# A new order for four engines around TensorE's fixed list of products, in linear attention and two MLPs on one core

## The reference

```python
# q, k, v: 8 x 8 heads x 576 x 64
q_s = softmax(q, axis=-1); k_s = softmax(k, axis=2)
x = q_s @ (k_s.T @ v)                       # -> 4608 tokens x 512
h = x @ w_in                                # 512 -> 2048
x2 = (max(h, 0) + alpha * min(h, 0)) @ w_out          # 2048 -> 512
h = x2 @ w_in2                              # 512 -> 1024
sm = exp(h - max(h)) / (sum(exp(h - max(h))) + 1e-9)
solu = h * sm
ln = (solu - mean) / sqrt(var + 1e-6) * g_ln
out = ln @ w_out2                           # 1024 -> 512
```

## Time and profile before

| what | value |
|---|---|
| median of 3 runs | 1277.55 us (1273.79 to 1279.27) |
| the profiled execution's own time | 1275.84 us |
| its span | 1274.0 us |
| mean granted clock of TensorE | 0.982 |
| bytes moved | 225 MB, 177 GB/s |

### The profile page before, as it was taken

One profiled execution on the slowest core, in us unless ns is written; L12 is line 12 of the kernel. 1 busy time (PEld: TensorE's weight loads), 2 busy tenths in 40 slices (PEclk: granted clock), 3 DMA queues, 4 the chain that ended last, 5 costly groups with the idle time before them and its releaser, 6 DMA issues.

```text
span 1274.0 us, 16162 instructions
## 1 busy us (share of the span) xinstructions
PE 1207.0 (95%) x6013; PEld 992.4 (78%) x6013; DVE 938.5 (74%) x1165; ACT 539.0 (42%) x744; POOL 306.8 (24%) x233
## 2 busy tenths in 40 slices
PE   7999999999999999999999999899898998998987
PEld 6778878878788888888888888877676776776765
DVE  7858778677663658777687777847878778778773
ACT  4433443434433435344444434434534534534432
POOL 5632413314131000000000001455144244244100
PEclk8999999999999999999999999999999999999999
DMA  9787787787956463452706335964434334334243
GB/s 238 228 250 257 236 255 241 232 274 231 292 191 211 150 234 105 153 177 67 243 22 208 122 100 182 267 195 136 146 121 155 122 118 156 123 116 157 91 147 118
DMA packets 211918, 225.07 MB, mean 177 GB/s; under 512 B 63208, under 2 KB 148224, under 8 KB 211712
## 3 DMA queue, kind: packets, MB, share of 16 engines
q1 hardware_dynamic: 206064, 212.50, 52.9%
q0 software_dynamic: 5728, 11.53, 3.0%
q10 hardware_dynamic: 48, 0.01, 0.0%
HBM read 128.51 MB, written 95.48 MB: 176 GB/s over the span
## 4 chain that ended last, share of the span: by engine, by line
PE 71%; DVE 13%; issue 5%; DMA 5%; POOL 2%; SPq 2%; ACT 1%; DVEq 0%; POOLq 0%; ACTq 0%
PE ps_y L1812 8%; PE ps_y L1814 8%; PE ps_y L1813 8%; PE ps_y L1898 5%; PE ps_y L1902 5%; PE ps_y L1900 5%; DVE e L1639 5%; PE ps_y L1956 3%; PE ps_y L1957 3%; PE ps_y L1958 3%; PE ps_m L1898 3%; PE ps_m L1902 3%; PE ps_m L1900 3%; PE ps_m L1748 2%; DVE zl L1648 2%
## 5 line engine op out<-in xcount | busy, mean ns | idle before, releaser
L1812 PE MATMUL ps_y<-X,W 128*128 128x512 f32 x576 | 227.4, 395 | 0.0
L1813 PE MATMUL ps_y<-X,W 128*128 128x512 f32 x576 | 225.0, 391 | 0.0
L1814 PE MATMUL ps_y<-X,W 128*128 128x512 f32 x576 | 224.9, 391 | 0.0
L1340 DVE SCALAR_TENSOR_TENSOR gst<-gst,nslope,ps_y 128x512 f32<-128x512 f32 x144 | 104.5, 732 | 114.9 <-ACT gst L952 114.6
L952 ACT ACTIVATE gst<-ps_y 128x512 f32<-128x512 f32 x144 | 85.8, 596 | 225.2 <-PE ps_y L1814 174.4
L1956 PE MATMUL ps_y<-WO,zh 128*128 128x512 f32 x288 | 120.0, 417 | 43.5 <-DVE zl L1648 43.5
L1812 PEld LDWEIGHTS ps_y<-X,W 128*128 128x128 f32 x576 | 108.4, 188 | 23.3
L1814 PEld LDWEIGHTS ps_y<-X,W 128*128 128x128 f32 x576 | 108.5, 188 | 23.1
L1813 PEld LDWEIGHTS ps_y<-X,W 128*128 128x128 f32 x576 | 108.6, 188 | 22.0
L1898 PE MATMUL ps_y<-rh,WOc 128*128 128x512 f32 (+1 forms) x320 | 118.0, 369 | 0.0
L1900 PE MATMUL ps_y<-rl,WOc 128*128 128x512 f32 (+1 forms) x320 | 117.9, 368 | 0.0
(11 more groups left out here) (189 smaller groups left out, 2587.2 us busy)
## 6 DMA issues: line engine op xcount, KB each, us to landing
g_scratch<-gst SPq DMA_DIRECT2D x144, 256.0 KB, 3.5
RX<-g_scratch SPq DMA_DIRECT2D x36, 512.0 KB, 3.6
z_scratch<-zb SPq DMA_DIRECT2D x36, 512.0 KB, 2.7
zt<-z_scratch SPq DMA_DIRECT2D x144, 128.0 KB, 2.8
ws_scratch<-whl SPq DMA_DIRECT2D x22, 512.0 KB, 4.4
RY<-g_scratch SPq DMA_DIRECT2D x18, 512.0 KB, 4.6
RZ<-g_scratch SPq DMA_DIRECT2D x18, 512.0 KB, 4.6
x2r<-x_scratch SPq DMA_DIRECT2D x18, 512.0 KB, 4.6
```

The lines of the kernel that those rows point to most:

```text
L1812: nc.tensor.matmul(o, W1[:, f, 0, a, :], x[:, 0, a, :], start=(a == 0), stop=False)
L1813: nc.tensor.matmul(o, W1[:, f, 0, a, :], x[:, 1, a, :], start=False, stop=False)
L1814: mm = nc.tensor.matmul(o, W1[:, f, 1, a, :], x[:, 0, a, :], start=False, stop=(a == KT - 1))
```

## The change

TensorE's list is not touched. The other four lists are.

- **GpSimd.** In the periods n = 5 to 14 the order is: both powers of n - 2, a wait for P3 of n, the sums for n + 2, a wait for P6 of n, the low part for n + 1. Before it was powers, low part, sums, with no wait for TensorE. The first and last periods have orders of their own, without these waits.
- **DVE.** In those periods norm_tile(n - 2, 0) stands ahead of form_u and norm_tile(n - 2, 1) ahead of form_v; tile_max(n - 1, 0) ahead of form_12 and form_21. In the third product's last unit, v and c22 stand behind both b_low of k = 4, where they stood between them.
- **ACT.** out_copy(n - 3, 0) goes from the middle to the end of the period's list, zt_high(n - 2, 0) ahead of the exponentials, h11_copy between them.
- **SP.** store_out(n - 3, 0) now stands between the store and the load of z(n - 2, 1), store_out(n - 4, 1) between the store and the load of z(n - 2, 0).
- The periods 0 to 4 and from 15 on are written out in new orders on all four.

```diff
--- before.py
+++ after.py
@@ -705,38 +705,66 @@
...
-            for n in range(5, PERIODS + 4):
-                if n - 4 < PERIODS:
-                    store_out(n - 4, 1)
-                if n - 2 < PERIODS:
-                    store_z(n - 2, 0)
-                    load_z(n - 2, 0)
-                if n - 3 < PERIODS:
-                    store_out(n - 3, 0)
-                if n - 2 < PERIODS:
-                    store_z(n - 2, 1)
-                    load_z(n - 2, 1)
-                if n + 3 < PERIODS:
-                    load_x2(n + 3)
+            for n in range(5, 15):
+                store_z(n - 2, 0)
+                store_out(n - 4, 1)
+                load_z(n - 2, 0)
+                store_z(n - 2, 1)
+                store_out(n - 3, 0)
+                load_z(n - 2, 1)
+                load_x2(n + 3)
+            store_out(11, 1)
+            store_z(13, 0)
+            load_z(13, 0)
+            store_z(13, 1)
+            store_out(12, 0)
+            load_z(13, 1)
...
+            store_z(15, 0)
+            load_z(14, 1)
+            load_z(15, 0)
+            store_out(13, 0)
...
+            store_out(15, 0)
+            store_z(17, 0)
+            load_z(17, 0)
+            store_out(15, 1)
+            store_out(16, 0)
+            store_z(17, 1)
+            load_z(17, 1)
+            store_out(16, 1)
+            store_out(17, 0)
+            store_out(17, 1)
@@ -852,6 +880,10 @@
                 nc.gpsimd.tensor_tensor(x2l[n % 2][:, :, :], x2[n % 2][:, :, :], x2h[n % 2][:, :, :].bitcast(F32),
                                         ALU.subtract).then_inc(x2l_ok, 1)
 
+            def after_block(n, count):
+
+                pool.wait_ge(m1_done, PARTS * n + count)
+
             def power(n, t):
                 pool.wait_ge(var_ok, 2 * n + t + 1)
                 nc.gpsimd.tensor_tensor(st[:, t, 8:9], st[:, t, 7:8], mhalf[:, :], ALU.pow).then_inc(rstd_ok, 1)
@@ -866,27 +898,40 @@
             load_wo2(1)
             x2_low(1)
             x2_sums(2)
-            x2_low(2)
             x2_sums(3)
             power(0, 0)
+            x2_low(2)
             x2_low(3)
             x2_sums(4)
             power(0, 1)
             x2_low(4)
+            power(1, 0)
             x2_sums(5)
-            power(1, 0)
             power(1, 1)
             x2_low(5)
             x2_sums(6)
             power(2, 0)
             power(2, 1)
-            for n in range(5, PERIODS + 2):
+            for n in range(5, 15):
                 power(n - 2, 0)
                 power(n - 2, 1)
-                if n + 1 < PERIODS:
-                    x2_low(n + 1)
-                if n + 2 < PERIODS:
-                    x2_sums(n + 2)
+                after_block(n, 3)
+                x2_sums(n + 2)
+                after_block(n, 6)
+                x2_low(n + 1)
+            power(13, 0)
+            power(13, 1)
+            x2_sums(17)
+            x2_low(16)
+            power(14, 0)
+            power(14, 1)
+            x2_low(17)
+            power(15, 0)
+            power(15, 1)
+            power(16, 0)
+            power(16, 1)
+            power(17, 0)
+            power(17, 1)
 
 
         @block.scalar
@@ -1152,61 +1197,101 @@
             first_copy(0)
             h11_copy(0)
             exp_tile(0, 0)
+            first_copy(1)
+            square_tile(0, 0)
             x2_high(2)
-            first_copy(1)
             exp_tile(0, 1)
...
-            for n in range(5, PERIODS + 4):
-                if n - 2 < PERIODS:
-                    square_tile(n - 2, 1)
-                if n < PERIODS:
-                    first_copy(n)
-                if n - 4 < PERIODS:
-                    out_copy(n - 4, 1)
-                if n - 3 < PERIODS:
-                    zt_high(n - 3, 1)
-                if n + 1 < PERIODS:
-                    x2_high(n + 1)
-                if n - 3 < PERIODS:
-                    out_copy(n - 3, 0)
-                if n < PERIODS:
-                    h11_copy(n)
-                if n - 2 < PERIODS:
-                    zt_high(n - 2, 0)
-                if n - 1 < PERIODS:
-                    exp_tile(n - 1, 0)
-                    exp_tile(n - 1, 1)
-                    square_tile(n - 1, 0)
+            for n in range(5, 15):
+                out_copy(n - 4, 1)
+                first_copy(n)
+                square_tile(n - 2, 1)
+                zt_high(n - 3, 1)
+                x2_high(n + 1)
+                zt_high(n - 2, 0)
+                exp_tile(n - 1, 0)
+                h11_copy(n)
+                exp_tile(n - 1, 1)
+                square_tile(n - 1, 0)
+                out_copy(n - 3, 0)
+            square_tile(13, 1)
+            out_copy(11, 1)
+            first_copy(15)
+            x2_high(16)
+            exp_tile(14, 0)
+            zt_high(12, 1)
+            out_copy(12, 0)
+            zt_high(13, 0)
+            h11_copy(15)
+            exp_tile(14, 1)
+            square_tile(14, 0)
+            first_copy(16)
+            zt_high(13, 1)
+            square_tile(14, 1)
+            exp_tile(15, 0)
+            x2_high(17)
...
 
 
         @block.vector
@@ -1563,14 +1648,9 @@
             for t in UNITS:
                 if t.r >= EARLY:
                     b_low(t)
-                if t.u == LAST_U and t.k == 4:
-                    if t.j == 0:
-                        post("v", t.u)
-                        post("c22", t.u)
-                    continue
                 if t.u == LAST_U and t.k == 5:
                     b_turn(UNITS[number(t.u, 4, t.j)])
-                if t.k in (0, 1, 2, 4):
+                if t.k in (0, 1, 2) or t.k == 4 and t.u < LAST_U:
                     b_turn(t)
                 if t.j == t.steps - 1:
                     if t.k == 0 and t.u > 0:
@@ -1648,68 +1728,124 @@
                 nc.vector.tensor_tensor(z_blocks(zl[:, t, :]), z_source(t), z_blocks(zh[:, t, :].bitcast(F32)),
                                         ALU.subtract).then_inc(zl_ok, 1)
 
-            def form_early(n):
-                form_u(n)
-                form_v(n)
-                form_22(n)
-
-            form_early(0)
+            form_u(0)
+            form_v(0)
+            form_22(0)
             form_12(0)
             tile_max(0, 0)
             form_21(0)
+            tile_solu(0, 0)
+            form_u(1)
+            form_v(1)
+            norm_tile(0, 0)
+            form_22(1)
             tile_max(0, 1)
-            tile_solu(0, 0)
-            form_early(1)
-            norm_tile(0, 0)
             form_12(1)
+            tile_solu(0, 1)
             form_21(1)
...
-            for n in range(5, PERIODS + 3):
+            for n in range(5, 15):
                 zt_low(n - 3, 0)
-                if n < PERIODS:
-                    form_early(n)
-                if n - 2 < PERIODS:
-                    norm_tile(n - 2, 0)
-                    norm_tile(n - 2, 1)
+                norm_tile(n - 2, 0)
+                form_u(n)
+                norm_tile(n - 2, 1)
+                form_v(n)
+                form_22(n)
                 zt_low(n - 3, 1)
-                if n < PERIODS:
-                    form_12(n)
-                    form_21(n)
-                if n - 1 < PERIODS:
-                    tile_max(n - 1, 0)
-                    tile_max(n - 1, 1)
-                    tile_solu(n - 1, 0)
-                    tile_solu(n - 1, 1)
+                tile_max(n - 1, 0)
+                form_12(n)
+                form_21(n)
+                tile_max(n - 1, 1)
+                tile_solu(n - 1, 0)
+                tile_solu(n - 1, 1)
+            zt_low(12, 0)
+            norm_tile(13, 0)
+            norm_tile(13, 1)
+            form_u(15)
+            tile_max(14, 0)
+            form_v(15)
+            tile_max(14, 1)
+            form_22(15)
+            zt_low(12, 1)
+            form_12(15)
+            tile_solu(14, 0)
+            zt_low(13, 0)
+            tile_max(15, 0)
+            form_21(15)
+            tile_solu(14, 1)
+            norm_tile(14, 0)
+            zt_low(13, 1)
...
+            zt_low(15, 1)
+            tile_solu(17, 0)
+            tile_max(17, 1)
+            zt_low(16, 0)
+            norm_tile(17, 0)
+            tile_solu(17, 1)
+            zt_low(16, 1)
+            norm_tile(17, 1)
+            zt_low(17, 0)
+            zt_low(17, 1)
 
 
```

138 lines of the change are left out of this document (107 added, 31 removed).

## The result

| kernel | median us | lowest to highest | ratio to before, 95% interval |
|---|---|---|---|
| before, measured beside it | 1278.2 (4 runs) | | |
| the change | 1222.97 (4 runs) | 1219.75 to 1224.71 | 0.9571 [0.9541, 0.9602] |

The change takes 4.3% off; 1222 was forecast. Its profiled execution took 1223.14 us, span 1221.3, mean clock 0.992.

A forecast was written before the change was run, and what follows sets the result against it. TensorE, 95% busy, was taken as the bound, losing 3.55 us per steady period to late zl and slow clock. 1275.84 - 35.4 - 0.4 - 1.0 - 18.5 = 1220.5, on the median 1222 us; range 1212 to 1240.

The forecast's parts named there:

- Steady periods: Periods n = 5 to 14: TensorE waits for nothing, 20.4 us each, 204.1 against 239.5: -35.4 us, bounds 0 to +14.
- The walk: New order followed through a steady period, offsets from P1's start: VectorE closes below 20.4 us with 2 us idle.
- The priced collisions: Left per steady period: a norm or zt_low beside the sums, 0.5 to 0.7 us; first solu behind x2_low's last 0.6.
- Last unit: Third product's last unit: TensorE waits 0.6 instead of 3.6 us, but x2_low(1) comes forward too: -0.4 us, bounds -4 to +2.
- TensorE waits there for what it won ahead of it: Third product's last unit: x2_low(1), 827.5 to 831.5, meets the last b_low at 828.4, so TensorE's won time is waited there.
- Head: Periods n = 0 to 4: 80.5 us before, walked to 75.3 or 79.0 plus slow clock: -1.0 us, bounds -6 to +4.
- The race: Head: x2_low(2) and norm(0,0) tie at 853.19; called for GpSimd, which costs 3.7 us more than VectorE winning.
- Tail: From P1(15): zt_low(12,1) 1 us late for M1, later zl ahead; 99.5 against 118.0: -18.5 us, bounds -1 and +10.
- A: Steady periods: x2_low or the sums catch another VectorE instruction, 21.5 us of VectorE per period; 1236 us, chance 0.14.
- B: Head and tail: seven tight margins slip and the head's race is lost; 1234 us, chance 0.08.
- C: Steady periods: another loop (P1 to h11, z's round trip through memory) keeps them near 23 us; 1250 to 1256, chance 0.04.
- D: Steady periods: x2 lands late, x2_low(n+1) becomes the period's end, 26.5 us each; slower, 1295 us, chance 0.03.

## Why the prediction was right, step by step

- **Steady periods, -35.4 forecast, -35.4 measured.** The walk holds in its offsets too. The sums were to start 7.6 us behind P1: they start at 7.6 (1006.74). x2_low from 13.9: 13.84. The first L1708 at 17.3: 17.27. zt_low(n-3,1) by 11: 10.4. VectorE's idle time was put at 2 us and is 3.0. The priced collisions came: L1708 lost 0.45 us where 0.6 were set, and zt_low and the sums held each other in turn.
- **What the steady step left out** is why. It credited the placement of x2_low behind P6. The runs show the same period of 20.4 (from n = 6 on) with GpSimd's old order, and without the two waits, and that VectorE's order alone gives 27 of the 35 us with the collision in place. The mechanism was right, that the time lost was the norm held by x2_low, but its cure was drawn too narrow: I followed one path to the norm and did not ask which of the edits was needed for it.
- **Last unit, -0.4 forecast with bounds -4 to +2, +2.7 measured**, outside them in this profile, +1.1 to +1.4 in five others. The step that failed is "TensorE waits there for what it won ahead of it". Both collisions are where it put them. But 3.35 us of wait (3.6 in the forecast) became 0.62 + 0.20 + 4.26 = 5.08, +1.7: TensorE and VectorE come sooner, while ACT's x2_high(1), which stands ahead of the last b_high, still waits for the sums. That is 1.3 of the 4.26 us, as the run with the later x2_low(1) shows, and the walk did not have it in the way. The slow clock, no term of the sum either, costs 2.0 us here and some 1.6 in before (120 matmuls from 820.08 to 836.05 that start 0.12 apart at full clock). Most of what is left stands at the edges of two more gaps: a row lasts 0.28 us where matmuls start 0.12 apart, and a wait counts from the row's end.
- **Head, -1.0 forecast, +0.9 measured**, well inside -6 to +4. The walk's own 79.0 us against 80.5 would have been -1.5, so the term is half a microsecond off its working. The race was called for GpSimd and fell to it, by 0.06 us, in this profile; the wait at P6(1) is 6.47 us (3 or 7 forecast). In other profiles with the same head it fell to VectorE (the runs with GpSimd's old order and with the old last unit: a wait of 2.8 us), so the call was no better than a guess between two outcomes. That these 3.6 us are part of the 5 us by which executions of the change differ is likely, but was not shown. The later waits, 1.59 at P6(2) and 0.68 at P1(5), are not named in the prediction. And TensorE is busy there for 72.4 us, as in before (72.5), against the 69.4 of bare work: 3 us, where 1 was set for slow clock.
- **Tail, -18.5 forecast, -18.2 measured.** The wait of 1.1 us was put at M1(12) and came at the last M1, where zl(17,1) was to be ready 0.5 us early. It came 1.4 late, since zh of that tile waits for its load; ACT, then TensorE:

```profile
1209.19 1.06 ACT L1189 ACTIVATE zh<-zt 128x1024 fp32r<-128x1024 f32 x1 [6.27 <-DMA zt<-z_scratch]
...
1211.56 0.50 PE L2092 MATMUL ps_y<-WO,zh 128*128 128x512 f32 x1 [1.41 <-DVE zl L1728]
```

  The half microsecond of slow clock did not come (1.00 in the stretch of that wait).
- **The sum.** The two misses in the last unit and the head, +3.1 and +1.9, with the tail's +0.3, are 5.3 us against the profiled 1275.84; the 2.7 us by which this execution reached the last unit earlier hid half of them. So the profiled time was missed by 2.6 us where the steps missed by 5.3, or 0.4%; that the median came within 1 us of 1222 is in part luck. The bounds named step by step add up to 1211 to 1252 around 1222, wider than the 1212 to 1240 stated.
- **The rivals.** A (the collision only moves) did not come; of its x2_low only 0.45 us a period moved, onto L1708. B (head and tail give nothing) was right on the head and wrong on the tail. C and D had no sign: no other loop near 23 us, x2_low ends at 17.9 and the next P1 wants it at 20.4. The Trainium skill's rule (SBUF — State Buffer, Who interferes with whom) that the engine that issues first keeps the shared pair for its whole instruction agrees in both directions: L1719 4.44 and L1587 4.16 us behind x2_low, and a sum of 1.76 us behind zt_low.

## What to carry to other kernels

Before you credit one edit of several, run each alone on the old kernel and take each alone out of the new one: here either of two was enough to end the collision next to VectorE's new order, and the two added waits were worth nothing that could be measured. When you free an instruction, list everything queued behind the one that held it, on that engine and on the engines that wait for those: a wait taken away at one product came back with 6.45 of its 6.47 us two products later, and 3.7 of 4.9 us won in the last unit were lost because x2 landed no sooner and a one-column instruction stood behind the sums that waited for it, until that instruction was moved up. Read more than one profile of a kernel whose order holds a race: the same code gave waits of 4.26 or 2.94 us, and of 6.47 or 2.83. Price a wait of TensorE with the clock behind it.

## What the hardware showed that was not expected

- A wait of 4.26 us is followed by a granted clock of 0.50, the lower level, 1.2 GHz (831.45 to 835.50): 20 matmuls start 0.21 us apart instead of 0.12, and the unit pays 2.0 us. Behind waits of 2.94 us it pays 1.3 to 1.6. Behind a wait of 1.32 us, in the run with the later x2_low(1), the clock in the same 96 matmuls stayed at 1.00.
- Behind the same instruction (power) GpSimd's next one and VectorE's norm start within 0.06 us of each other, GpSimd's first: 853.06 against 853.12, and with the same lead in the runs without the two waits, with the later x2_low(1) and with form_22(1) first. In the run with the old last unit x2_low had to wait for ACT too, 0.3 us, and VectorE won.
- Beside x2_low VectorE's block transposition and its maxima keep their length (L1729 1.25 us from 852.09 in the run with the old last unit, L1699 1.21 us from 1014.95 in the change), while an instruction over two SBUF tensors (L1587, 4.16 us) or the norm over 1024 elements (L1719, 4.44 us) stands still until its end.
